# First-layer activation kept in its PSUM bank, its two halves split in the same step, and both attention slots behind the down group

## The reference, cut to what matters

```python
out_d = sm_attn(q_d, k_d, v_d)            # queries, keys, values averaged over 4 positions
scores = np.where(abs(pos_i - pos_j) < 4, scale * q @ k.T, -1e9)
x = np.repeat(out_d, 4, axis=2) + softmax(scores) @ v   # 4 x 576 tokens, 8 heads of 64
h = x @ w_in;  g = np.maximum(0.01 * h, h);  x = g @ w_out       # 2304 x 512 -> 2048 -> 512
h = x @ w_in2; g = h - np.tanh(h);           out = g @ w_out2    # 2304 x 512 -> 2048 -> 512
```

## Time and profile before

| what | value |
|---|---|
| median of 3 runs (lowest, highest) | 1002.15 us (1001.6, 1003.06) |
| the profiled execution's own time | 1001.37 us |
| its span, first to last instruction | 999.6 us |
| PE busy | 965.1 us, 97% |
| DVE, ACT, POOL busy | 585.8, 565.8, 410.4 us |
| granted PE clock, mean | 0.98; 1.00 in every stretch shown below |
| layer 1 with attention, tile 0 to 5 | about 72 to 481 us of the span |
| layer 1 alone, tile 6 and 7 | about 483 to 588 us |
| PE busy from 500 to 550 us of the span, in tile 6 and 7 | 50.00 us of 50.00 |

### The profile page before, as it was taken

How to read it: one execution, slowest core, us unless ns; L and a number is a source line. 1 busy time by engine, 2 the same in 40 slices (tenths; PEclk the granted TensorE clock), 3 DMA queues, 4 the chain that set the end, 5 groups by cost and what they waited for, 6 DMA issues and landing times.

```text
span 999.6 us, 19154 instructions
## 1 busy us (share of the span) xinstructions
PE 965.1 (97%) x6672; PEld 906.1 (91%) x6672; DVE 585.8 (59%) x1082; ACT 565.8 (57%) x1382; POOL 410.4 (41%) x341
## 2 busy tenths in 40 slices
PE   6888999999999999999999999999999999999998
PEld 6778999999999999999999988889899889898996
DVE  6466644653565456436424866676676676766764
ACT  3454554644554635546344767776576666766664
POOL 3346551723723616418162646633323233333232
PEclk9579999999999999999999999999999999999999
DMA  5653521121012102200200402100000000000000
GB/s 123 155 149 94 133 50 25 27 49 39 16 41 48 29 19 48 48 25 3 64 2 1 138 3 84 53 33 1 1 31 1 26 5 0 31 0 0 32 1 32
DMA packets 87220, 41.46 MB, mean 41 GB/s; under 512 B 59776, under 2 KB 80768, under 8 KB 87168
## 3 DMA queue, kind: packets, MB, share of 16 engines
q1 hardware_dynamic: 87168, 40.78, 15.4%
HBM read 36.04 MB, written 4.72 MB: 41 GB/s over the span
## 4 chain that ended last, share of the span: by engine, by line
PE 84%; DVE 5%; ACT 4%; POOL 2%; issue 2%; SPq 2%; DMA 1%; ACTq 0%; DVEq 0%
PE ph L460 12%; PE ph L462 12%; PE ph L461 12%; PE acc L536 6%; PE acc L537 6%; PE acc L538 6%; PE acc L489 6%; PE acc L490 6%; PE acc L491 6%; PE banks L370 3%; PE banks L388 2%; DVE g_lo L855 2%; PE banks L376 2%; PE banks L364 1%; PE banks L396 1%
## 5 line engine op out<-in xcount | busy, mean ns | idle before, releaser
L1022 POOL TENSOR_TENSOR g_lo<-scratch,g_hi 128x384 fp32r<-128x384 f32 x96 | 125.8, 1311 | 258.9 <-ACT g_hi L656 258.9
L870 DVE TENSOR_TENSOR g<-g,ph 128x288 f32<-128x288 f32 x128 | 57.9, 453 | 191.5 <-ACT g L676 191.1
L992 POOL TENSOR_TENSOR in_lo<-w_whole,in_hi 128x512 fp32r<-128x512 f32 x64 | 83.4, 1304 | 161.7 <-ACT in_hi L640 161.1
L460 PE MATMUL ph<-x_hi,w_hi_a 128*128 128x288 f32 (+1 forms) x448 | 143.9, 321 | 1.9 <-DVE x_lo L850 1.9
L462 PE MATMUL ph<-x_hi,w_lo_a 128*128 128x288 f32 (+1 forms) x448 | 140.4, 313 | 0.0
L461 PE MATMUL ph<-x_lo,w_hi_a 128*128 128x288 f32 (+1 forms) x448 | 140.3, 313 | 0.0
L676 ACT ACTIVATE g<-ph 128x288 f32<-128x288 f32 x128 | 52.4, 410 | 153.3 <-PE ph L462 151.8
L906 DVE SCALAR_TENSOR_TENSOR scratch<-scratch,ph 128x384 f32<-128x384 f32 x96 | 53.2, 554 | 111.4 <-ACT scratch L721 106.8
L997 POOL TENSOR_TENSOR out_lo<-w_whole,out_hi 128x512 fp32r<-128x512 f32 x64 | 86.4, 1350 | 58.8 <-ACT out_hi L644 58.2
L720 ACT ACTIVATE scratch<-ph 128x384 f32<-128x384 f32 x96 | 46.8, 487 | 108.4 <-PE ph L462 106.8
L855 DVE TENSOR_TENSOR g_lo<-g,g_hi 128x288 fp32r<-128x288 f32 x128 | 88.0, 687 | 2.7 <-ACT g_hi L656 2.7
(11 more groups left out here) (166 smaller groups left out, 2740.6 us busy)
## 6 DMA issues: line engine op xcount, KB each, us to landing
out_dram<-o_stage SPq DMA_DIRECT2D x18, 256.0 KB, 2.1
w_whole<-in_moe_w_in_dram SPq DMA_DIRECT2D x16, 256.0 KB, 4.4
w_whole<-in_moe_w_out_dram SPq DMA_DIRECT2D x16, 256.0 KB, 4.2
qn<-in_q_dram SPq DMA_DIRECT2D x28, 144.0 KB
kn<-in_k_dram SPq DMA_DIRECT2D x28, 144.0 KB
v4n<-in_v_dram SPq DMA_DIRECT2D x28, 144.0 KB
vw<-in_v_dram SPq DMA_DIRECT2D x28, 122.5 KB
scratch<-in_moe_w_in_dram SPq DMA_DIRECT2D x8, 256.0 KB, 2.8
```

The source lines that it names most:

```text
L460: pe.matmul(bank, whi, x_hi[:, c, 0:width], start=(c == 0), stop=False)
L992: pool.tensor_tensor(in_lo[:, f % 2, :], w_whole[:, f - KEPT, 0:DM], in_hi[:, f % 2, :].bitcast(F32), ALU.subtract).then_inc(in_lo_done, 1)
L1022: pool.tensor_tensor(g2_lo[:, f % 3, :], g2[:, f % 2, :], g2_hi[:, f % 3, :].bitcast(F32), ALU.subtract).then_inc(g_lo_done, 1)
```

## The change

Three edits in layer 1:

- DVE's maximum is written back into the PSUM bank `ph1` and no longer into `g1`. `split_g` and `lo_of_g1` read it from there.
- `split_g` and `lo_of_g1` of step `f` move from step `f + 1` into step `f`, behind slot `2f`. So `hidden1(f)` must wait for `g_lo_done` of `f - 2`, since the bank is read until then, and the leak of `f` waits for `g_done` of `f - 2` only.
- PE plays slot `2f` behind `down1(f - 2)`, together with slot `2f + 1`.

```diff
 def hidden1(tile, f):                                       # PE
-                wait_from(pe, g_done, n - 1)
+                wait_from(pe, g_lo_done, n - 1)
 def layer1(...):                                            # PE
                         hidden1(tile, f)
-                    between(2 * f)
                     if ahead and f == CF + LAG1 - 1:
                         hidden1(tile + 1, 0)
                     if f >= LAG1:
                         down1(tile, f - LAG1)
+                    between(2 * f)
                     between(2 * f + 1)
 def layer1(...):                                            # ACT
                         act.wait_ge(h_done, n + 1)
-                        wait_from(act, g_lo_done, n - 1)
+                        wait_from(act, g_done, n - 1)
...
-                    if f:
-                        split_g(n - 1, f - 1, g1[:, (f - 1) % 2, :], g1_hi)
                     between(2 * f)
+                    if f < CF:
+                        split_g(n, f, ph1[:, f % 2, 0:T1], g1_hi)
 def lo_of_g1(n, f):                                         # DVE
-                dve.tensor_tensor(g1_lo[:, f % 3, :], g1[:, f % 2, :], g1_hi[:, f % 3, :].bitcast(F32),
+                dve.tensor_tensor(g1_lo[:, f % 3, :], ph1[:, f % 2, 0:T1], g1_hi[:, f % 3, :].bitcast(F32),
 def layer1(...):                                            # DVE
-                        dve.tensor_tensor(g1[:, f % 2, :], g1[:, f % 2, :], ph1[:, f % 2, 0:T1], ALU.max)\
+                        dve.tensor_tensor(ph1[:, f % 2, 0:T1], g1[:, f % 2, :], ph1[:, f % 2, 0:T1], ALU.max)\
...
-                    if f:
-                        lo_of_g1(n - 1, f - 1)
                     between(2 * f)
+                    if f < CF:
+                        lo_of_g1(n, f)
```

## The result

| | kernel before | changed kernel |
|---|---|---|
| median (lowest, highest) of 16 runs each | 1002.61 us (1000.2, 1004.84) | 1005.81 us (1003.73, 1008.15) |
| ratio to before, 95% interval | 1 | 1.0035 (1.0025 to 1.0044) |
| span of the profiled execution | 999.6 us | 1002.0 us |

The change makes the kernel slower by 0.35%, 3.2 us between the medians. The forecast said slower, 1007. Its sum, though, was +5.1, and one term of +3.9 is not in the trace at all. Smaller terms that I had too low fill part of the gap. The profiled executions took 1001.37 us before and 1003.73 after, so the traces can account for 2.4 of the 3.2.

The account below looks back on a forecast made before the run. PE, busy 97% of the span, plus its stalls was taken as the bound. The terms summed to +5.1 on the profiled 1001.37, so 1006.5, stated as 1007 us; own range 1004.5 to 1009.5, 8 in 10 within 1000 to 1010.

Parts of the forecast that it names:

- R2: Rival: L817 is served ahead of POOL's L997, so down1(11) waits for nothing; no change, 1003.4 us; chance 0.24.
- Stall (a): Layer step 3: transposes L376 lose 0.49 to POOL's late L976; goes, -2.4 in five tiles; tile 0's 2.32 idle, -2.0.
- Stall (b): Layer step 12: the next transposes' wait for L976, 0.25 a tile, goes; -1.4 over six tiles.
- fewer switches: Mixed tiles: merging adjacent attention groups saves 0.06 a pair, nine pairs, about 0.5 a tile; -3.1 in six.
- Steps 3' and 4': Attention steps in layer step 8: new PE stall on ACT's copy that down1(6) had hidden; +0.68 a tile, +4.1 in six.
- steps 14 and 15: Attention steps in layer step 5: new PE stall on ACT's copy L620; net +0.39 a tile, +2.3.
- POOL's queue: Layer steps 8 to 11: later POOL splits delay softmax and out_lo(11), so down1(11) waits 0.6 to 0.65; +3.9 in six tiles.
- Tile end: The g_lo wait goes but x split and out_lo(15) come later; +0.6 in tiles 1 to 4, +0.5 in tile 0, +2.9.
- Tiles 6 and 7: Tiles 5 and 6, without attention at their end, +0.2 together; tile 7, where POOL starts later, +0.6 (-1 to +2).
- Price nothing: hidden1(f) waiting for g_lo of f - 2 costs nothing; nearest at step 3, where lo(1) ends some 0.8 early.
- R1: Rival: at the tile end the g_lo wait goes and nothing replaces it, 4.5 gained; faster, 999.9 us; chance 0.16.
- R3: Rival: in_lo(12), out_lo(10) and in_lo(13) are late too, 0.6 more a tile; slower still, 1011 us; chance 0.10.

Follow-up runs that it names:

- the step alone: Kernel before with both roundings of the activated tile moved into the same step, tile still in SBUF, PE's order as before: 1001.35 us, ratio 0.9984.
- The fastest version: Changed kernel with slot 2f ahead again in steps 5, 8, 15; in tiles 6 and 7 weights rounded first, accumulators kept behind the first rounding: 991.47 us, ratio 0.9886.
- the version with the tile in SBUF: Changed kernel with the maximum writing g1 in SBUF again and both roundings reading it, still in the same step, PE's order as changed: 1015.43 us, ratio 1.0141.
- PE's order alone: Kernel before with only slot 2f moved behind the down group; tile in SBUF and roundings one step later stay: 1008.56 us, ratio 1.0073.
- three exceptions a tile: Changed kernel, but in layer steps 5, 8 and 15 PE plays slot 2f ahead of the down group again: 993.78 us, ratio 0.9927.
- the bank alone: Kernel before with the activated tile in PSUM, both roundings still one step later and PE's order as before: 1007.5 us, ratio 1.0058.
- the bank with the earlier step: Changed kernel with PE's order of before, slot 2f ahead of the down group; tile in PSUM and same-step roundings stay: 998.38 us, ratio 0.9966.

## Why the prediction was right, and where it was wrong

The side was right, but partly by luck: the largest term behind it did not happen. Without that term the same sum is +1.2, or 1003.4, which is rival R2's figure, and which the prediction itself called no change. The measured time lies 2.4 above it. Most of what fills the gap in the traces is in tile 7 (1.1 more than forecast), in tile 0 from `hidden1(3)` on (-0.69, where the terms other than POOL's add up to -1.2) and in tile 6 (0.25 more). By its own terms, for the mixed tiles:

- **Stall (a)**: -0.49 a tile forecast, -0.52 measured. In tile 0 the stretch with the 2.32 stall is 1.95 shorter; forecast 2.0. Confirmed.
- **Stall (b) and fewer switches**: -0.23 and -0.5 a tile forecast, and 0.27 + 0.41 + 0.13 = 0.81 measured in the three rows of the table that hold them. Right in sum, less so in its parts: hidden groups 7, 8 and 14 come 0.05 to 0.08 earlier each, as the 0.06 a pair that I worked out, but 0.35 lies in one stretch, to hidden group 15, where attention steps 15 and 16 merge. By the starts in tile 2, 0.15 of it is step 15's last group (L396, 0.66 before to the down group behind it, 0.51 now to step 16), 0.14 the down group (1.82 before, 1.68 now) and 0.07 the hidden group (1.75 and 1.68). So a switch out of L396 costs more than the ones that I had measured; why is not shown.
- **Steps 3' and 4'**: +0.68 forecast, +0.86 measured; **steps 14 and 15**: +0.39 and +0.37. PE's idle time ahead of L396 is 0.23 each there, though, not the 0.5 to 0.7 that I named as the sign. Mechanism right, the first size 0.18 low: 0.10 of it stands in the rows above (1.06 in place of 0.96), and another 0.10 is step 4' itself, which starts 1.13 ahead of `hidden1(9)` where it started 1.03 ahead before.
- **POOL's queue**: +3.9 forecast, 0 measured. This is the step that failed, see below.
- **Tile end**: +0.6 forecast, +0.84 - 0.28 = +0.56 measured in tiles 1 to 4.
- **Tiles 6 and 7**: +0.1 and +0.6 forecast, +0.35 and +1.68 measured. The mechanism in tile 7 was named (ACT waits for the maximum before it rounds weights), but I charged it at one down group, and it holds at four in a row, about 0.5 each. "Price nothing" for the added wait of `hidden1(f)` was wrong here: `hidden1(2)` of tiles 6 and 7 is late by 0.26, because the accumulators are kept ahead of the first rounding. In the step alone, where `hidden1(f)` still waits for the maximum, that stretch is as before (0.01). The fastest version, which keeps the accumulators behind the rounding, has 0.01 there too, and its tile 6 gave back 0.33.

For tiles 1 to 4 the forecast without POOL's term is +0.45 each, and the trace has +0.42.

**The step that failed.** The claim, counted against `hidden1(9)`, was that POOL reaches `out_lo(11)` 0.95 later and PE reaches `down1(11)` 0.6 earlier, so that a margin of 0.95 becomes a wait of 0.6 to 0.65. In tile 2, against the start of `hidden1(9)`, `down1(11)` starts 0.58 earlier, as forecast, but `out_lo(11)` ends only 0.17 later. The margin shrank from 0.95 to 0.20 and held. So PE's side was right, and POOL's delay was 0.8 too long. About half of that is ahead of softmax: L992 for step 10 starts 1.52 later against `hidden1(8)` (1.5 forecast) but 0.66 later against `hidden1(9)` (0.9 forecast), since the longer stall at step 8 delays `hidden1(9)` too, and attention's subtraction L817 ends 0.57 later (0.9 forecast). Then the chain made up 0.4: from L817's end to POOL's product L976 it is as long as before (4.49 and 4.51), but from the start of L976 to the end of `out_lo(11)` it takes 4.60 in place of 5.03. The rows of DVE around POOL's product, first of the kernel before, then of the changed kernel:

```profile
258.81 0.99 DVE L855 TENSOR_TENSOR g_lo<-g,g_hi 128x288 fp32r<-128x288 f32 x1
259.72 1.20 DVE L836 TENSOR_SCALAR rs<-rs 96x3 f32<-96x3 f32 x1
```
```profile
259.14 0.70 DVE L836 TENSOR_SCALAR rs<-rs 96x3 f32<-96x3 f32 x1
...
259.96 0.42 DVE L855 TENSOR_TENSOR g_lo<-ph,g_hi 128x288 fp32r<-128x288 f32 x1
```

And POOL's product, before and after:

```profile
259.44 1.46 POOL L976 TENSOR_TENSOR pl<-pl,rs 128x630 f32<-128x630 f32 x1
...
263.19 1.28 POOL L997 TENSOR_TENSOR out_lo<-w_whole,out_hi 128x512 fp32r<-128x512 f32 x1
```
```profile
259.77 1.25 POOL L976 TENSOR_TENSOR pl<-pl,rs 128x630 f32<-128x630 f32 x1
...
262.22 0.90 POOL L981 TENSOR_TENSOR pd<-pd,rs 96x432 f32<-96x432 f32 x1
263.08 1.29 POOL L997 TENSOR_TENSOR out_lo<-w_whole,out_hi 128x512 fp32r<-128x512 f32 x1
```

In the change `lo` stands behind attention's work, so L836 runs before POOL's product and not beside it; L976 and L981 are each 0.2 shorter (L981 took 1.13 before). That comes from where the subtraction stands, not from the bank: the version with the tile in SBUF has 1.25 and 0.91 as well, and PE's order alone, with the old place, 1.46 and 1.11. I had carried the durations of contended instructions from the old trace into a layout in which they no longer met. With them the margin of 0.20 would be a wait of about 0.2, an estimate from these rows, so this explains half of the miss and not all of it. The version with the tile in SBUF shows how near it was: there `down1(11)` does wait in every mixed tile. R2 gave the outcome (no wait), but not for its reason, since L817 began 0.28 behind L997 and was again done 0.67 behind its end. R1 and R3 did not happen: the x split started 0.85 later, where R1 asked for 0.1 at most, and the splits that R3 feared were in time.

**Tile 0's start.** From `hidden1(3)` on, tile 0 is 0.69 shorter than before. Ahead of it, PE's granted clock was lower in the changed kernel's profile for longer. The windows of the stretch from 68 to 80 us, in the changed kernel and then in that of before: PE's busy time, its clock as a share of full speed, DMA.

```profile
68.00:80.00 12.00, 11.25 (x55) 0.57 0.88 262
```
```profile
68.00:80.00 12.00, 9.90 (x94) 0.86 0.75 225
```

In the changed kernel PE ran most of that stretch at 1.2 GHz; before, most of it at 2.4. The stretch moves from kernel to kernel: the start of tile 1 lies between 138.86 and 144.37 in the eleven profiles, in no order that follows the edits. This is why I compare tiles and not spans. What moves it is not settled.

## What to carry to other kernels

Playing two small groups together saves a switch (here 0.06 us) only if the second doesn't read what another engine makes of the first; if it does, the large group between them was hiding that round trip (here 0.9 to 1.06 us), so merge group by group and not by rule: three exceptions a tile turned +0.35% into -0.7%. A buffer held longer is free only if its last reader is moved forward with it: the bank alone cost 0.6%, the bank with the earlier step gained 0.3%, about half of it by the earlier step alone. And when a margin of a microsecond decides a term worth four, lay the chain out with undisturbed durations as well as those of the old trace, count both of its sides from the same event, and give both ends a chance.

## What the hardware showed that I had not expected

DVE's subtraction with two SBUF inputs can wait for several POOL instructions in a row. In the version with the tile in SBUF, DVE at the tile's layer step 12 and POOL beside it:

```profile
269.49 4.18 DVE L855 TENSOR_TENSOR g_lo<-g,g_hi 128x288 fp32r<-128x288 f32 x1 [1.51 <-ACT g_hi L656]
```
```profile
268.73 0.91 POOL L981 TENSOR_TENSOR pd<-pd,rs 96x432 f32<-96x432 f32 x1
269.59 1.29 POOL L997 TENSOR_TENSOR out_lo<-w_whole,out_hi 128x512 fp32r<-128x512 f32 x1
270.84 1.28 POOL L992 TENSOR_TENSOR in_lo<-w_whole,in_hi 128x512 fp32r<-128x512 f32 x1
272.08 1.28 POOL L997 TENSOR_TENSOR out_lo<-w_whole,out_hi 128x512 fp32r<-128x512 f32 x1
```

An instruction of 0.45 us took 4.18. It began while L981 still ran, and ended 0.31 behind the last of the three splits, each of which began behind it. These POOL instructions were not slowed. It does not always go so: in the same trace the subtraction that began at 266.25 took 1.37 and ended 0.31 behind POOL's L976 (266.06, 1.25 long), and it was POOL's next split (267.26) that took 1.50 in place of 1.28. What decides between the two is not shown. The same subtraction with one input from PSUM averaged 0.451, over 128 of them in the changed kernel, with POOL as busy (404.3 us against 406.1).

The Trainium skill, "SBUF — State Buffer", section "Who interferes with whom", says that a DVE instruction with two SBUF inputs contends with a POOL instruction that reads SBUF and one with at most one SBUF input does not. The traces agree with this (means of 793 to 809 ns in the two versions with the earlier step and the tile in SBUF, 451 in PSUM). It also says that the order of issue decides who blocks. The rows above do not agree with that: by the records DVE's instruction stood ahead of three POOL splits and was blocked through all of them.
